# The opening of a fused token-mixing kernel: the first group's attention as four terms that TensorE turns and sums, and the loads ahead of it put in another order

## The reference

```python
# 1. attention over 7 taps, 8 heads of 24 channels
w = exp(weight_gen - max); w = w / (sum(w) + 1e-9)          # [B, S, 8, 7]
out[b, s, h, g] = sum_k w[b, s, h, k] * x_pad[b, s + k, h, g]
# 2. channel mixing
xk = mu_k * x + (1 - mu_k) * x_prev;  xr = mu_r * x + (1 - mu_r) * x_prev
k = relu(xk @ w_k); v = (k * k) @ w_v; r = sigmoid(xr @ w_r); x = r * v
# 3. gated projection, with a 3-tap convolution over tokens
h = relu(x @ w_in); conv = sum_j conv_w[j] * hp[:, j:j+S, :]
out = (h * sigmoid(conv)) @ w_out
```

## Time and profile before

| | |
|---|---|
| median of 3 runs | 723.04 us (722.88 to 723.24) |
| the profiled execution | 723.3 us, of which 721.5 us are the span from its first to its last instruction |
| busy, whole span | PE 703.1, DVE 673.5, ACT 630.2 us |
| first `att_mult` of group 0 | at 9.27 us |
| first `mix_k` (group 0) | at 21.75 us |
| first useful matmul of group 0 | at 22.82 us |

### The profile page before, as it was taken

One profiled execution on the slowest core, in us unless ns is written; L12 is line 12 of the kernel. 1 busy time (PEld: TensorE's weight loads), 2 busy tenths in 40 slices (PEclk: granted clock), 3 DMA queues, 4 the chain that ended last, 5 costly groups with the idle time before them and its releaser, 6 DMA issues.

```text
span 721.5 us, 10642 instructions
## 1 busy us (share of the span) xinstructions
PE 703.1 (97%) x3556; PEld 601.9 (83%) x3556; DVE 673.5 (93%) x991; ACT 630.2 (87%) x1272; POOL 3.6 (0%) x12
## 2 busy tenths in 40 slices
PE   5889999999999999999999999999999999999997
PEld 5777778888888888888888888888888888888997
DVE  7998999989999999989999999989999899887788
ACT  3789797979999797989999798989979798998986
POOL 1000000000000000000000000000000000000000
PEclk9999999999999999999999999999999999999999
DMA  5711010100202010010201001020101002000000
GB/s 143 252 56 55 1 55 1 56 22 1 78 0 78 1 55 22 16 63 0 77 1 56 22 9 70 1 77 1 55 23 56 22 1 73 0 23 1 23 14 36
DMA packets 9067, 28.81 MB, mean 40 GB/s; under 512 B 1310, under 2 KB 3896, under 8 KB 8886
## 3 DMA queue, kind: packets, MB, share of 16 engines
q1 hardware_dynamic: 8856, 28.12, 11.6%
q10 hardware_dynamic: 158, 0.03, 0.0%
HBM read 21.75 MB, written 6.39 MB: 39 GB/s over the span
## 4 chain that ended last, share of the span: by engine, by line
PE 82%; DVE 10%; issue 3%; ACT 2%; DMA 1%; SPq 1%; DVEq 0%; ACTq 0%
PE up L337 36%; PE od L442 22%; PE dn L404 4%; PE dn L420 4%; PE dn L423 4%; PE dn L424 4%; PE dn L427 4%; PE dn L426 3%; DVE att L1715 2%; DVE prod L1703 2%; PE mid L308 2%; DVE kq_lo L1779 1%; DMA h<-in_moe_w_k 1%; DVE cv L1827 1%; DVE cv L1814 1%
## 5 line engine op out<-in xcount | busy, mean ns | idle before, releaser
L442 PE MATMUL od<-wo_sb,gat 128*128 128x192 f32 x1040 | 182.2, 326 | 1.6 <-ACT o_sb L929 1.0
L442 PEld LDWEIGHTS od<-wo_sb,gat 128*128 128x128 f32 x1040 | 172.7, 190 | 8.6 <-DVE gat L1836 1.3
L1779 DVE TENSOR_TENSOR kq_lo<-ksq,kq_hi 128x512 fp32r<-128x512 f32 (+2 forms) x136 | 89.7, 661 | 17.6 <-ACT kq_hi L875 17.3
L1814 DVE SCALAR_TENSOR_TENSOR cv<-h,prm,cv 128x512 f32<-128x512 f32 (+1 forms) x136 | 96.8, 723 | 5.4 <-ACT cv L911 4.4
L1827 DVE SCALAR_TENSOR_TENSOR cv<-h,prm,cv 128x512 f32<-128x512 f32 (+1 forms) x136 | 97.9, 721 | 0.1
L911 ACT ACTIVATE cv<-h,prm 128x512 f32<-128x512 f32 (+1 forms) x136 | 94.1, 695 | 1.9 <-DVE gat L1836 1.4
L900 ACT ACTIVATE h<-up 128x512 f32<-128x512 f32 (+2 forms) x136 | 77.8, 573 | 19.6 <-PE up L337 17.2
L1715 DVE TENSOR_TENSOR att<-att,prod 128x768 f32<-128x768 f32 (+1 forms) x102 | 94.6, 927 | 0.4
L1703 DVE TENSOR_TENSOR prod<-xin,wgt 128x768 f32<-128x768 f32 (+1 forms) x102 | 93.3, 928 | 0.5
L1836 DVE TENSOR_TENSOR gat<-h,cv 128x512 f32<-128x512 f32 (+1 forms) x136 | 88.4, 661 | 1.5 <-ACT cv L918 1.2
L859 ACT ACTIVATE ksq<-up 128x512 f32<-128x512 f32 (+2 forms) x136 | 78.3, 576 | 11.3 <-PE up L337 9.1
(11 more groups left out here) (110 smaller groups left out, 1334.0 us busy)
## 6 DMA issues: line engine op xcount, KB each, us to landing
xin<-in_x SPq DMA_DIRECT2D x14, 960.0 KB, 4.7
out<-o_sb SPq DMA_DIRECT2D x16, 384.0 KB, 2.3
wgt<-in_weight_gen SPq DMA_DIRECT2D x1, 1092.0 KB, 11.0
xin<-in_x SPq DMA_DIRECT2D x1, 864.0 KB, 4.7
h<-in_moe_w_v SPq DMA_DIRECT2D x1, 768.0 KB, 4.8
wo_sb<-in_moe_w_out SPq DMA_DIRECT2D x1, 768.0 KB, 12.4
h<-in_moe_w_k SPq DMA_DIRECT2D x1, 512.0 KB, 5.3
h<-in_moe_w_k SPq DMA_DIRECT2D x2, 256.0 KB, 6.5
```

Of the source, the lines that this page charges most:

```text
L442: mm = nc.tensor.matmul(o, tile[:, b * P:(b + 1) * P], wo_sb[:, c, :], start=(c == 0 and b % 2 == 0), stop=(c == NC - 1), skip_group_check ...
L1779: nc.vector.tensor_tensor(ring(kq_lo, c, n), ring(ksq, c, n), ring(kq_hi, c, n).bitcast(F32), ALU.subtract).then_inc(kql_ok, 1)
L1814: nc.vector.scalar_tensor_tensor(o, win(w, c, -1), prm[:, 3 + c:4 + c], o, ALU.mult, ALU.add)\
```

## The change

**The attention of group 0** is held as four terms: taps 0 and 1, taps 2 and 3, tap 4, taps 5 and 6. The first tap of a term is written straight into the term's tile, and the second added to it. So three sums stay on DVE (taps 1, 3 and 6) and three go. Terms 0 and 1 lie in `gat`, term 2 in `prod2`, term 3 in `att`. TensorE multiplies each term by the identity, as a plain matmul which turns it, and accumulates all four in `mid0` and `mid1`. ACT doubles the 64 channels of each term.

**Loads.** SP issues `w_k` ahead of the five parameter loads, no longer waits for `w_k`, and goes straight on to x for group 1, `w_v` and the rest. The six `w_r` transfers move to ACT's own queue, behind its early sigmoid and ahead of `cast_wk`.

**Warming transposes.** 30 ahead of the wait for the parameters, 14 behind it (64 before, all behind it), and 17 where 23 stood. They write `od1`, and the parameters are turned into `od0`, so `t_part` no longer waits for `prm_ok` (the first `down2` does).

```diff
+        TERMS = {0: ((0, 1), (2, 3), (4,), (5, 6))}
...
+        def term_tile(g, j):
+
+            n = (1 + size(g) if eq(g, 0) else size(g)) * AW
+            if j == len(TERMS[g]) - 1:
+                at = 0 if eq(g, 0) else AW
+                tile = att[:, at:at + n]
+            elif j < 2:
+                tile = gat[:, j * 4 * AW:j * 4 * AW + n]
+            else:
+                tile = prod[2][:, 0:n]
+            return tile.rearrange("p (q c) -> p q c", c=AW)
...
             for a, b in HALO_RUNS:
                 sp.dma_start(xin[a:b, 0:TAPS * D], before(x_flat, a, b, TAPS, D)).then_inc(x_in, 16)
+            load_up_weights(sp, w_k, 0, wk_in)
...
-            load_up_weights(sp, w_k, 0, wk_in)
-
-            sp.wait_ge(wk_in, 48)
-            for c0, c1, at in ((0, D, 0), (P, D, D)):
...
+            def summed(dst, src, begin, end):
+
+                for n in range(src.shape[1]):
+                    mm = nc.tensor.matmul(dst[:, n * P:(n + 1) * P], src[:, n, :], ident[:, :],
+                                          start=(begin and n == 0), stop=end, skip_group_check=True)
+                return mm
+
+            def term_part(g, j, part):
+                if part == 1:
+                    eng_wait_term(pe, g, j)
+                else:
+                    pe.wait_ge(dbl_ok, terms_before(g) + j + 1)
...
+            def double_term(g, j):
+                v = term_tile(g, j)
+                eng_wait_term(act, g, j)
+                nc.scalar.activation(v[:, :, D:AW], v[:, :, P:D], ACT.Copy).then_inc(dbl_ok, 1)
...
                 exps(0)
                 cast_wk()
+                double_term(0, 0)
                 cast_wr()
+                double_term(0, 2)
+                double_term(0, 1)
                 double(0)
...
             pe.wait_ge(id_ok, 2)
+            warm(30)
             pe.wait_ge(prm_in, 16 * 5)
...
-            warm(64)
+            warm(14)
             first_steps()
-            for i in range(3, NG - 5):
+            for i in range(4, NG - 5):
                 step(i)
```

More of the change, by code:

```diff
@@ L185, in n_windows, with attn_adds, first_taps, term_of @@
             return w - 1
+        TERMS = {0: ((0, 1), (2, 3), (4,), (5, 6))}
+        def attn_adds(g):
+            return sum(TAPS - len(TERMS.get(q, (0,))) - 1 for q in range(g))
+        def first_taps(g):
+            return [t[0] for t in TERMS[g]]
+        def term_of(g, k):
+            return [j for j, t in enumerate(TERMS[g]) if k in t][0]
+        def adds_before(g, k):
+            return sum(1 for q in range(k) if q not in (first_taps(g) if g in TERMS else (0,)))
+        def term_tile(g, j):
[8 more added lines that the diff above has]
+            return tile.rearrange("p (q c) -> p q c", c=AW)
         def wgt_rows(lo, hi):
@@ L233, in load_up_weights, with terms_before, eng_wait_term @@
             eng.dma_start(raw_w(i + 1, D2, P), w[P:D, :]).then_inc(arrived, 16)
+        def terms_before(g):
+            return sum(len(TERMS[q]) - 1 for q in TERMS if q < g)
+        def eng_wait_term(eng, g, j):
+            t = TERMS[g][j]
+            if len(t) > 1:
+                eng.wait_ge(at_add, attn_adds(g) + adds_before(g, t[-1]) + 1)
+            else:
+                eng.wait_ge(at_mul, (TAPS - 1) * g + t[0] + 1)
         @block.sync
@@ L310, in transposes @@
                 mm.then_inc(done, 1)
+            def summed(dst, src, begin, end):
[6 more added lines that the diff above has]
+                    eng_wait_term(pe, g, j)
+                else:
+                    pe.wait_ge(dbl_ok, terms_before(g) + j + 1)
+                if j == 0 and not eq(g, 0):
+                    if part == 1:
+                        pe.wait_ge(xk_ok, g)
+                        pe.wait_ge(xr_ok, g)
+                    else:
+                        pe.wait_ge(x2_ok, g)
+                summed(mid[part - 1], term_tile(g, j)[:, :, (part - 1) * P:part * P], j == 0, False)\
+                    .then_inc(term_t, 1)
             def t_part(g, part):
@@ L536, in first_steps @@
                 down2(1, 3)
+                down2(1, 4)
+                up2(2, 0)
+                up2(2, 1)
+                up2(2, 2)
+                down2(1, 5)
+                up2(2, 3)
+                up2(2, 4)
+                up2(2, 5)
+                down2(1, 6)
+                up2(2, 6)
+                up2(2, 7)
+                up1(3, 0)
+                up1(3, 1)
+                up1(3, 2)
+                r_part(3, 1)
+                up1(3, 3)
+                r_part(3, 2)
+                up1(3, 4)
+                up1(3, 5)
+                down1(3, 0)
+                down1(3, 1)
+                down1(3, 2)
+                up1(3, 6)
+                down2(1, 7)
+                t_part(4, 1)
+                down1(3, 3)
+                up1(3, 7)
+                t_part(4, 2)
+                down1(3, 4)
+                down1(3, 5)
+                down2(2, 0)
+                down1(3, 6)
+                down1(3, 7)
+                down2(2, 1)
+                down2(2, 2)
+                down2(2, 3)
             def step(i):
@@ L1695, in att_mult @@
                         dve.wait_ge(at_ok, g)
[L1696 to L1698 removed]
+                if g in TERMS:
+                    n = adds_before(g, k)
+                    if k not in first_taps(g) and n >= 2:
+                        dve.wait_ge(at_add, attn_adds(g) + n - 1)
+                elif k >= 4:
+                    dve.wait_ge(at_add, attn_adds(g) + k - 3)
                 x = xin[:, x0 * D:(x0 + nb) * D].rearrange("p (q h c) -> p q h c", q=nb, h=HEADS)
@@ L2180, in first_steps @@
                 att_add(6, 2)
+                xr_lo_part(5, 2)
+                att_mult(6, 3)
+                att_mult(6, 4)
+                att_add(6, 3)
+                conv_before(4, 2)
+                conv_before(4, 3)
+                conv_after(4, 1)
+                k_lo(5, 0)
+                gate(4, 0)
+                att_mult(6, 5)
+                k_lo(5, 1)
+                att_add(6, 4)
+                k_lo(5, 2)
+                att_mult(6, 6)
+                att_add(6, 5)
+                conv_after(4, 2)
+                att_add(6, TAPS - 1)
+                k_lo(5, 3)
+                conv_after(4, 3)
+                conv_before(4, 4)
+                gate(4, 1)
+                k_lo(5, 4)
+                conv_after(4, 4)
+                k_lo(5, 5)
+                softmax_back(7)
+                mix_r(6)
+                k_lo(5, 6)
+                gate(4, 2)
+                k_lo(5, 7)
+                mix_k(6)
+                conv_before(4, 5)
+                gate(4, 3)
+                gate(4, 4)
+                att_mult(7, 0)
+                y_mult(5, 1)
+                y_mult(5, 2)
+                conv_before(4, 6)
+                conv_after(4, 5)
+                y_lo_part(5, 1)
+                y_lo_part(5, 2)
+                conv_before(4, 7)
+                xr_lo_part(6, 1)
+                conv_after(4, 6)
+                gate(4, 5)
+                conv_after(4, 7)
+                att_mult(7, 1)
+                mix_2(6)
+                x_lo(6, 1)
+                gate(4, 6)
+                att_mult(7, 2)
+                gate(4, 7)
+                x_lo(6, 2)
+                conv_before(5, 0)
+                att_add(7, 1)
+                conv_before(5, 1)
+                conv_after(5, 0)
+                att_add(7, 2)
             def step(i):
```

145 lines of the change are left out of this document (121 added, 24 removed).

## The result

The changed kernel takes 724.55 us, median of 11 runs (723.93 to 725.58), against 723.08 us (722.88 to 723.24, 11 runs) of the kernel before: a ratio of 1.0022, 95% interval 1.0015 to 1.0030. It is 1.5 us slower where 2.4 us less were forecast. Eight of the 11 executions took 723.93 to 724.91 us, with a mean clock of 0.997 or 0.998; the other three took 725.34 to 725.58, with 0.994 or 0.995. The profiled one, at 724.12 us, is of the eight, and no trace shows one of the three.

What follows compares the result with a forecast made beforehand. PE bounds the body; in the opening DVE's sums and the `w_r` load run nearly level. 2.01 + 0.40 = 2.41 us from DVE, nothing for ACT, `w_r`, PE: 723.04 - 2.4 = 720.6 us, range 720.0 to 722.9 us.

Steps and rivals of the forecast that it cites:

- What bounds the kernel, and the slide: Opening sets the body's start; PE fills 77 to 680 us; work of 21.75 to 77 us slides whole, cost 0.
- DVE: Opening: three sums save 2.01 us, an ended wait for `w_r` 0.40; `mix_k` at 19.34 us.
- The `w_r` load, called the unknown: Opening, ACT's queue: last issue about 10.9 us, landing taken as 14.5 us, free until 15.1 us.
- an estimate of 16.1 us: `w_r` landing if queues switch by whole packets, gain 1.4 us; mechanism of the late-`w_r` rival, chance 0.17.
- PE is the step that failed: Opening: 14 transposes and 18 products behind the parameters, 3.7 us, ready at 16.8 us ahead of 17.07; no cost.
- the price: One identity product on PE in the opening: taken as 0.116 us, upper bound 0.163 us.
- the clock, which was a rival with a chance of 0.15: Opening: PE slow after a pause up to 3.2 us, or late with products; costs 0.9 to 1.4 us; chance 0.15.
- the row of the 1.5 us pause: Profile row before the change: PE stands 1.5 us ahead of 19.48 us and comes back at full speed.
- the rivals: `w_r` late 0.17; PE slow or late 0.15; change not doing what it says 0.06; slower 0.06.
- the end of the other sign: Slower case: `w_r` starved on ACT's queue by SP's backlog, up to 728.9 us, chance 0.06.
- The sign "products at 0.23 us up to 19 us": Opening, PE: named, beside an ACT wait for `w_r` beyond 15.1 us, as what would show the forecast wrong.

Runs made afterwards that it cites:

- e8: Changed kernel with all five parameter loads on ACT's queue ahead of `w_r` and the term parts reordered on PE: 721.20 us, ratio 0.9974.
- e1: Changed kernel with 62 instead of 30 warming transposes ahead of the wait for the parameters: 722.93 us, ratio 0.9998.
- e10: e1 with its 14 transposes behind the parameters made plain float32 products of the identity with the identity: 724.51 us, ratio 1.0019.
- e7: Changed kernel with 46 instead of 30 warming transposes ahead of the parameters: 722.65 us, ratio 1.0000.
- e3: Kernel before with the changed kernel's loads, 62 warming transposes ahead of the parameters and 40 behind: 723.54 us, ratio 1.0008.
- e4: Changed kernel with the loads of the kernel before, 30 warming transposes ahead of the parameters and 24 behind: 725.30 us, ratio 1.0026.
- e2: Changed kernel with the five parameter loads ahead of the `w_k` loads again on SP's queue: 723.34 us, ratio 1.0001.
- e5: e1 without the 14 warming transposes behind the parameters: 721.81 us, ratio 0.9981.
- e6: e1 with three terms, taps (0,1), (2,3,4), (5,6), so six products fewer and one sum more: 721.93 us, ratio 0.9985.

## Why the prediction was wrong

**What bounds the kernel, and the slide:** right. Span less `mix_k` is 699.8 us before and after.

**DVE:** right. 2.01 us for three sums and 0.40 for the wait; the last sum came 2.29 us sooner, 16.38 for 18.67, and e8 shows `mix_k` at 19.37 when nothing else holds it.

**The `w_r` load, called the unknown:** the landing came as forecast, 14.5 us, and by luck. The timeline of ACT and its queue:

```profile
5.95 0.36 ACTq L1102 DMA_DIRECT2D h<-in_moe_w_r  x1
...
7.96 0.20 ACT L1095 ACTIVATE early<-ident 128x1 f32<-128x1 f32 x1
...
8.68 0.62 ACTq L1104 DMA_DIRECT2D h<-in_moe_w_r  x1
...
14.62 0.42 ACT L1113 ACTIVATE wr_hi<-h 128x256 fp32r<-128x256 f32 x1
```

ACT cast `w_r` at 14.62 us without a wait; in e1 it waited for it until 14.46. But the issues began at 5.95 us, beside the early sigmoid and its table load, and not behind them at 8.04, so the last went out at 8.68 and not at 10.9. And each transfer took 6.0 to 6.8 us from issue to landing, where the forecast left 3.6 for the last one. The two errors cancelled. The rule of whole packets between two queues from the Trainium skill ("DMA: Bandwidth & Descriptors", queues, rings and completion order) led the prediction to an estimate of 16.1 us. The landing didn't bear this out, but its 16.1 - 10.9 = 5.2 us from issue to landing is nearer to the measured 6.0 than the forecast's 3.6. No trace shows how the queues share. `w_k` was cast from 12.45 us on, against 12.4 forecast.

**PE is the step that failed**, in two terms and in how they were put together. First the price: "above, what a plain float32 matmul with 192 columns does, 5.20 / 32 = 0.163 us". The 32 are instructions, and two of them are one product; the down products (L442) are 65 slots by 8 chunks, 520 products, and part 5 of the page counts 1040 (x1040, then the busy us and the mean ns of one):

```profile
L442 PE MATMUL od<-wo_sb,gat 128*128 128x192 f32 x1040 | 182.2, 326 | 1.6 <-ACT o_sb L929 1.0
```

So a product with 192 columns takes 0.325 us, and one with 128 takes 0.22 to 0.23 (the terms at full clock, e10). My upper bound was below the true value. 18 products at 0.107 us more are 1.9 us, and the last term, twice as long, adds 0.28 on the way to `zk`: 2.2 us.

Second the clock, which was a rival with a chance of 0.15. It came true in all 11 executions. The pause was 3.98 us and not "up to 3.2", since the transposes ahead of it were done at 9.07 us; the fall cost 0.68 us in the 14 transposes and 0.93 in the first term, 1.6 us. The medians agree: e1 is 1.6 us below the changed kernel, and in e7 a fall costs 1.9. The Trainium skill's rule ("TensorE: Matmul & The Clock Gate", Part 1) that an idle PE goes back to the lower level was the better guide than the row of the 1.5 us pause.

Third, the rivals were priced one at a time. Either alone stays in the range: e7's seven executions at full clock, where only the price is at work, have a median of 722.4 us, and the fall alone would give an estimated `mix_k` at 18.7 + 1.6 = 20.3 us and 721.6 us. The two add up on one chain: 19.34 + 0.12 (later start) = 19.46; PE's own chain without either would give 18.7; 18.7 + 2.2 + 1.6 = 22.5 us, and `mix_k` is at 22.49. I had 1.4 us as the worst for either and none for both, and put the end of the other sign into `w_r`. The sign "products at 0.23 us up to 19 us" did appear, but it meant half clock: the products from 17.79 us on took 0.22 us at a granted clock of 1.00.

## What to carry to other kernels

Before a price is taken from a row, count the instructions of the row against the operations in the program: here a plain float32 matmul is two, a transpose one. Work that is handed to an engine off the critical path starts when that engine is free of all that stands ahead of it in its queue; here 14 idle transposes and a wait for parameters stood ahead of 24 products. And a load that is moved behind another moves each wait for it, with the pause and the clock that go with it: order the parts by when each operand comes, and fill the pause (e8).

## What the runs showed of the hardware

- A plain float32 product of 128x128 with 128 columns takes 0.22 to 0.23 us and stands as two instructions in the profile; a transpose of the same size takes 0.113 to 0.116 us and stands as one (e1, e10).
- How short a pause harms PE's clock varies from execution to execution, told by a mean clock of 0.998 or less: 3.98 us took it down in 11 of 11, 2.44 us in 4 of 11, 1.84 us in 1 of 11 (e3), 1.31 and 2.16 us with 12 instructions between in 6 of 10 (e4), 0.92 and 1.52 us with six between in 6 of 11 (e2). No pause (e1) or none over 0.85 us (e5, e6, e8) did in 0 of 41. The kernel before, with 1.5 us behind unbroken work, doesn't show it in any of the 89 executions beside these runs.
- The fall isn't at the pause. In the changed kernel the granted clock still reads 1.00 up to 14.0 us, a microsecond behind the pause's end, then about 0.50 up to 17.5 us.
- ACT's queue issues transfers ahead of activations that stand before them in the program, and while ACT loads a table. The first `w_r` issue is at 5.95 us and the sigmoid ahead of it in the program at 7.96; its table load runs from 6.67 to 7.95 us, and issues start at 6.91 and 7.55.
- Beside SP's backlog the six `w_r` transfers on ACT's queue took 6.0 to 6.8 us from issue to landing; with the queues to themselves they took 2.0.
